# Moving the last expert's third output take one cosine step later, and another order of five small and middle-sized buffers

## The chip, the core and the metric

The kernel runs on one core of one Trainium2 chip. The metric is the device time of one launch in microseconds (us). One core has TensorE (PE, the matrix products; PEld is its weight load), VectorE (DVE), ScalarE (ACT), GpSimd (POOL) and SyncE (SP), which here only issues the loads and the stores. Each engine works through its own list of instructions; where one needs another's result, it waits on a counter (a semaphore).

## What is computed

A windowed attention, then a mixture of four experts, then a feed-forward block with a cosine in it:

```python
scores = q @ k.T / sqrt(D); mask: 0 <= i - j < 64; attn = softmax(scores); x = attn @ v
p = domain_probs / sum(domain_probs)
out = sum over e in 0..3 of p[:, e:e+1] * (relu(x @ w1[e]) @ w2[e])
h = out @ w_in;  g = h * cos(h);  result = g @ w_out
```

There are 1152 tokens of width 512. Each expert has 1024 hidden columns, the last block 2048, worked as two halves of 1024. All is float32.

## The kernel before

**Numbers in two parts.** Every operand of a large product is split into a high and a low part (`x_hi`, `x_lo`, `w_hi`, `w_lo`, `hp_hi`, `hp_lo`), and each product is three matmuls: high by high, high by low, low by high. ACT writes the high parts, DVE the low parts of activations, POOL the low parts of weights.

**Tiles.** Tokens are worked in three tiles of 384 (`TOK`, `NTOK = 3`), hidden columns in eight chunks of 128 (`FC = 8`). An *up* step of a chunk is 12 matmuls of 384 columns at L1153 (4 chunks of the width by 3 products). It reads weights as the stationary operand and x as the moving one, and writes one PSUM bank. A *down* step is 9 matmuls of 512 columns at L1181 (3 groups of 128 tokens by 3 products). It reads `hp_hi` or `hp_lo` as the stationary operand and weights as the moving one, and adds to the three PSUM banks 4, 5 and 6 (`y_ps[0:3]`) over the eight chunks. Experts 1 to 3 do two of their tiles in products of pairs (L1198, L1212, with helpers `t_hi`, `t_lo`, `ex_hi`, `ex_lo`), and the third tile alone with up and down steps.

**Taking outputs.** When all eight down steps of a tile are done, DVE empties the three banks into `acc`. For experts it multiplies by the tokens' shares: `pick_shares` copies three shares per partition from `p_tok` to `p_now` (L874), and `take_shared` does one 512-column instruction per bank (L882 for expert 0, L885 afterwards), each of which raises the counter `y_taken` by one. The first down step of the next tile waits for `y_taken` bank by bank: `down_cells(0, ...)` has `pe.wait_ge(y_taken, y_count(tile, c))` before the three matmuls of each c.

**From the experts to the cosine block.** After the third expert tile of expert 3 (`pe_alone(E - 1)`) PE's list is: up 0 of the cosine block, down 6 of the expert, up 1, down 7 (the last of the expert), up 2, and then, in `pe_turn`, up 3, down 0, up 4, down 1, up 5, down 2 and so on. Down 0 is the first that writes banks 4 to 6 again. Hidden chunks of the cosine block go through bank `f % 4`, and DVE and ACT turn each into h times cos(h) in this chain:

- ACT `cosine`: `c_u` from the bank (L692), then `hidden_high_cos` of the step before (L681), then for some steps `high_weights` (L608), then `c_abs` (L699) and `c_cos` (L701), which reads `half_pi`.
- DVE `times_cosine`: `c_k` (L978), `c_r1` (L980), `c_r2` (L983), `hidden_low_cos` of the step before (L863), then a take if the step has one, then `h_raw` = `c_cos` times the bank (L991).

The three steps 0, 1 and 2 before the turn are written out in a loop of their own (`for i in range(LAG)`, `LAG = 3`), on ACT and on DVE. In step 1 of it DVE also takes the expert's third tile, `take_last_of_experts`: one copy and three takes. POOL meanwhile works eight instructions of 128 columns per chunk of weights (L426).

**Buffers.** `sb(name, shape)` places buffers one behind another in each partition, each start rounded up to a multiple of 32 bytes. `half_pi` is one number per partition, `p_now` nine, `apart` sixteen that nobody reads or writes.

Of the kernel before, what the change touches and what calls it, by code (L numbers as in the profile page):

```python
# [26 lines left out]
P = 128  # L27
# [16 lines left out]
FC = F1 // P  # L44
TOK = 384
NTOK = N // TOK
OC = TOK // P
TILES = N // P
HALVES = F2 // F1
LAG = 3  # L50
# [58 lines left out]
def build(nc, q, k, v, probs, weights, out):  # L109
    with ExitStack() as ctx:  # L110
        def sb(name, shape, dt=F32):
            return ctx.enter_context(nc.sbuf_tensor(name, shape, dt))
# [7 lines left out]
        x_hi = sb("x_hi", [P, DC, N], F32R)  # L120
        x_lo = sb("x_lo", [P, DC, N], F32R)
        p_tok = sb("p_tok", [P, E, TILES])
        half_pi = sb("half_pi", [P, 1])

        sb("apart", [P, 16])
        hp_hi = sb("hp_hi", [P, HP, TOK], F32R)
        hp_lo = sb("hp_lo", [P, HP, TOK], F32R)
        h_raw = sb("h_raw", [P, HP, TOK])
        p_now = sb("p_now", [P, NTOK, OC])
        ident = sb("ident", [P, P])  # L130
        mask = sb("mask", [P, 3, P])
        zeros = sb("zeros", [P, P])
# [138 lines left out]
        MIX = NTOK + E - 1  # L271
# [528 lines left out]
        def _(dve):  # L800
# [60 lines left out]
            def hidden_low_cos(f, s):  # L861
                dve.wait_ge(hp_hi_done, s + 1 + C_HI)
                nc.vector.tensor_tensor(hp_lo[:, f % HP, :], h_raw[:, f % HP, :], hp_hi[:, f % HP, :],  # L863
                                        ALU.subtract).then_inc(hp_lo_done, 1)
# [109 lines left out]
            def times_cosine(f, s, late, take=None, which=()):  # L974
                n = s - MIX * FC
                bank_h = h_ps[f % HB][:, 0:TOK]
                dve.wait_ge(cos_u, n + 1)
                nc.vector.tensor_scalar_sub(c_k, c_u, ROUND).then_inc(cos_k, 1)  # L978
                dve.wait_ge(cos_k, n + 1)
                nc.vector.scalar_tensor_tensor(out=c_r1, in0=c_k, scalar=-TWO_PI_HI, in1=bank_h,  # L980
                                               op0=ALU.mult, op1=ALU.add).then_inc(cos_r1, 1)
                dve.wait_ge(cos_r1, n + 1)
                nc.vector.scalar_tensor_tensor(out=c_r2, in0=c_k, scalar=-TWO_PI_LO, in1=c_r1,  # L983
                                               op0=ALU.mult, op1=ALU.add).then_inc(cos_r, 1)
                if late:
                    hidden_low_cos((f - 1) % FC, s - 1)
                if take is not None:
                    take(*which)
                dve.wait_ge(cos_done, n + 1)
                dve.wait_ge(hp_hi_done, s - HP + 1 + C_HI)  # L990
                nc.vector.tensor_tensor(h_raw[:, f % HP, :], c_cos, bank_h, ALU.mult).then_inc(cos_taken, 1)  # L991

            def dve_turn(e, t, turn, last=False, inputs=False):
                for f in range(FC):
                    g, s = (f + LAG) % FC, turn * FC + f + LAG
                    if last and f >= FC - LAG:
                        if f == FC - LAG:
                            hidden_low_cos(FC - 1, s - 1)
                    elif f < FC - 1:
                        times_cosine(g, s, True)  # L1000
                    else:
                        times_cosine(g, s, True, take_outputs, (e, turn, t))
                    if inputs and f in TURNS:
                        next_input_low((t - 1) % NTOK * OC + TURNS.index(f))
                if last:
                    take_outputs(e, turn, t, last)
# [67 lines left out]
                    take_last_tile(E - 1, c)  # L1074

            for i in range(LAG):
                if i == 1:
                    times_cosine(i, MIX * FC + i, True, take_last_of_experts)
                else:
                    times_cosine(i, MIX * FC + i, i > 0)  # L1080
            dve_turn(E, 0, MIX, inputs=True)
            with dve.Fori(1, NTOK - 1) as t:
                dve_turn(E, t, MIX + t)
# [376 lines left out]
```

## Time and profile before

| | us |
|---|---|
| median of 3 runs | 645.05 |
| lowest, highest | 644.95, 645.10 |
| the profiled execution, its time | 645.05 |
| its span, first to last instruction | 643.0 |
| PE busy in the span | 632.9 |
| DVE, ACT, POOL busy | 306.4, 259.2, 269.6 |

The span leaves out 2.05 us around the instructions. Since the profiled execution took the median time, what is added to or taken from its span is added to or taken from 645.05. Matmuls overlap, so a matmul's own duration is longer than the distance from its start to the next one's start; where the text needs PE's pace, it takes starts.

### The profile page before, as it was taken

To read this page: it belongs to the slowest core of one execution; us is meant where nothing else is said; L and a number is where in the kernel's file an instruction comes from. 1 tells how busy PE (TensorE), PEld (TensorE's weight loads), DVE (VectorE), ACT (ScalarE), POOL (GpSimd) and SP (SyncE) were. 2 spreads that over 40 slices of the span, in tenths; PEclk is the share of its full clock that TensorE was granted. 3 is DMA by queue.
4 is the path that set the end of the run, shared out by engine and by line. 5 is a ranking of instruction groups with operands and counts; after the bars stand their busy time and mean duration, and the time that the engine had idled before them with its cause. 6 is when DMAs were issued, how large, how long until landed. Compare 5 with 4: busy or idle time off the path is not lost.

```text
span 643.0 us, 10145 instructions
## 1 busy us (share of the span) xinstructions
PE 632.9 (98%) x3656; PEld 564.9 (88%) x3656; DVE 306.4 (48%) x722; ACT 259.2 (40%) x554; POOL 269.6 (42%) x404
## 2 busy tenths in 40 slices
PE   7899999999999999999999999999999999999998
PEld 6687889999999999999999999999899999999996
DVE  6655331215433315433415333427775666756674
ACT  6685412233321233321233321246554467555452
POOL 6683336597730187730197730277100059400000
PEclk9999999999999999999999999999999999999999
DMA  9855200003210012210022120043100012001011
GB/s 280 260 185 143 104 1 1 1 19 113 66 67 1 1 65 65 65 65 0 1 65 66 66 66 1 2 128 102 34 0 1 0 41 93 1 0 49 0 50 49
DMA packets 21896, 37.25 MB, mean 58 GB/s; under 512 B 2784, under 2 KB 14048, under 8 KB 21856
## 3 DMA queue, kind: packets, MB, share of 16 engines
q1 hardware_dynamic: 20688, 36.71, 17.7%
q8 instruction: 24, 0.39, 0.2%
q10 hardware_dynamic: 1168, 0.02, 0.1%
q14 instruction: 16, 0.13, 0.1%
HBM read 34.36 MB, written 2.36 MB: 57 GB/s over the span
## 4 chain that ended last, share of the span: by engine, by line
PE 95%; DVE 2%; issue 1%; ACT 1%; POOL 0%; DVEq 0%
PE bank L1181 31%; PE bank L1153 31%; PE bank L1212 15%; PE bank L1198 14%; PE bank L1145 2%; PE bank L1109 1%; PE bank L1129 1%; DVE s_sb L823 1%; PE bank L1295 1%; PE bank L1334 1%; ACT prob L576 0%; DVE acc L972 0%; ACT x_hi L589 0%; DVE p_now L874 0%; DVE prob_t L838 0%
## 5 line engine op out<-in xcount | busy, mean ns | idle before, releaser
L426 POOL TENSOR_TENSOR w_lo<-w_raw,w_hi 128x128 fp32r<-128x128 f32 (+1 forms) x252 | 149.7, 628 | 208.8 <-ACT w_hi L608 206.7
L1153 PE MATMUL bank<-x_hi,w_hi 128*128 128x384 f32 (+1 forms) x384 | 132.2, 344 | 0.2 <-DVE x_lo L852 0.2
L1153 PE MATMUL bank<-x_hi,w_lo 128*128 128x384 f32 (+1 forms) x384 | 129.5, 337 | 0.0
L1153 PE MATMUL bank<-x_lo,w_hi 128*128 128x384 f32 (+1 forms) x384 | 129.1, 336 | 0.0
L1181 PE MATMUL bank<-w_hi,hp_hi 128*128 128x512 f32 x288 | 113.6, 394 | 0.3 <-DVE acc L882 0.3
L1181 PE MATMUL bank<-w_lo,hp_hi 128*128 128x512 f32 x288 | 113.9, 395 | 0.0
L1181 PE MATMUL bank<-w_hi,hp_lo 128*128 128x512 f32 x288 | 113.6, 394 | 0.0
L926 DVE TENSOR_TENSOR h_raw<-bank,h_raw 128x384 f32<-128x384 f32 x84 | 46.8, 557 | 97.2 <-PE bank L1198 97.2
L1153 PEld LDWEIGHTS bank<-x_hi,w_hi 128*128 128x128 f32 x384 | 72.2, 188 | 5.4 <-issue 1.0
L1153 PEld LDWEIGHTS bank<-x_lo,w_hi 128*128 128x128 f32 x384 | 72.2, 188 | 3.3
L632 ACT ACTIVATE hp_hi<-h_raw 128x384 fp32r<-128x384 f32 x48 | 25.3, 527 | 117.6 <-DVE h_raw L926 117.6
L857 DVE SCALAR_TENSOR_TENSOR hp_lo<-bank,hp_hi 128x384 fp32r<-128x384 f32 x48 | 26.5, 556 | 96.8 <-ACT hp_hi L640 54.8
L1153 PEld LDWEIGHTS bank<-x_hi,w_lo 128*128 128x128 f32 x384 | 72.0, 188 | 0.0
L1181 PEld LDWEIGHTS bank<-w_lo,hp_hi 128*128 128x128 f32 x288 | 54.0, 187 | 11.6
L1181 PEld LDWEIGHTS bank<-w_hi,hp_hi 128*128 128x128 f32 x288 | 54.1, 188 | 9.4 <-issue 0.6
L1181 PEld LDWEIGHTS bank<-w_hi,hp_lo 128*128 128x128 f32 x288 | 54.0, 188 | 8.7
L1212 PE MATMUL bank<-w_lo,hp_hi 128*128 128x512 f32 x144 | 56.4, 392 | 0.0
L1212 PE MATMUL bank<-w_hi,hp_lo 128*128 128x512 f32 x144 | 56.4, 391 | 0.0
L1212 PE MATMUL bank<-w_hi,hp_hi 128*128 128x512 f32 x144 | 56.3, 391 | 0.0
L699 ACT ACTIVATE c_abs<-c_r 128x384 f32<-128x384 f32 x48 | 25.3, 527 | 46.2 <-DVE c_r L983 46.1
L608 ACT ACTIVATE w_hi<-w_raw 128x1024 fp32r<-128x1024 f32 x40 | 42.0, 1050 | 0.0
L991 DVE TENSOR_TENSOR h_raw<-c_cos,bank 128x384 f32<-128x384 f32 x48 | 26.6, 553 | 32.4 <-ACT c_cos L701 32.4
(103 smaller groups left out, 965.9 us busy)
## 6 DMA issues: line engine op xcount, KB each, us to landing
w_raw<-in_weights SPq DMA_DIRECT2D x43, 512.0 KB, 3.6
q_t<-in_q SPq DMA_DIRECT2D x12, 192.0 KB, 4.6
result<-acc SPq DMA_DIRECT2D x9, 256.0 KB, 2.0
w_raw<-in_weights SPq DMA_DIRECT2D x8, 256.0 KB, 5.9
k_t<-in_k SPq DMA_DIRECT2D x8, 224.0 KB, 5.3
v_w<-in_v SPq DMA_DIRECT2D x4, 384.0 KB, 4.8
v_w<-in_v SPq DMA_DIRECT2D x4, 320.0 KB, 6.5
k_t<-in_k SPq DMA_DIRECT2D x4, 192.0 KB, 4.0
```

Source lines behind the costliest of these rows:

```text
L426: last = nc.gpsimd.tensor_tensor(w_lo[:, f, at:at + part], raw[:, at - begin:at - begin + part], w_hi[:, f, at:at + part], ALU.subtract)
L608: nc.scalar.activation(w_hi[:, f, :], w_raw[:, f % STAGE, :], ACT.Copy).then_inc(w_hi_done, 1)
L632: nc.scalar.activation(hp_hi[:, i, :], h_raw[:, i, :], ACT.Relu).then_inc(pair_hi_done, 1)
L699: nc.scalar.activation(c_abs, c_r2, ACT.Abs).then_inc(cos_abs, 1)
L857: nc.vector.scalar_tensor_tensor(out=hp_lo[:, f % HP, :], in0=ps[:, 0:TOK], scalar=0.0, in1=hp_hi[:, f % HP, :], op0=ALU.max, op1=ALU.subt ...
L926: nc.vector.tensor_tensor(h_raw[:, place, :], ps, h_raw[:, other, :], ALU.add).then_inc(pair_taken, 1)
L991: nc.vector.tensor_tensor(h_raw[:, f % HP, :], c_cos, bank_h, ALU.mult).then_inc(cos_taken, 1)
L1145: last = nc.tensor.matmul(o_bank(m)[heads, block_of * WIN:(block_of + 1) * WIN], v_w[:, r, WINDOW_OF[t][block_of], heads], prob_t[:, h, bl ...
L1153: last = nc.tensor.matmul(ps[:, 0:TOK], w[:, f, chunk(c)], x[:, c, token_cols(t)], start=c == 0 and i == 0, stop=c == DC - 1 and i == 2)
L1181: last = nc.tensor.matmul(y_ps[c][:, :], h[:, f % HP, chunk(c)], w[:, f, DM:2 * DM], start=f == 0 and i == 0, stop=f == FC - 1 and i == 2)
L1198: last = nc.tensor.matmul(bank[(g * PRODUCTS + j) % 2][:, 0:TOK], a, b, start=c == 0 and i == 0, stop=c == 1 and i == 2)
L1212: last = nc.tensor.matmul(pair_y[t][c][:, :], h[:, i, chunk(c)], w[:, f, DM:2 * DM], start=f == 0 and k == 0, stop=f == FC - 1 and k == 2)
```

## The change

```diff
@@ buffers
         x_lo = sb("x_lo", [P, DC, N], F32R)
         p_tok = sb("p_tok", [P, E, TILES])
-        half_pi = sb("half_pi", [P, 1])
-
-        sb("apart", [P, 16])
+        p_now = sb("p_now", [P, NTOK, OC])
         hp_hi = sb("hp_hi", [P, HP, TOK], F32R)
         hp_lo = sb("hp_lo", [P, HP, TOK], F32R)
         h_raw = sb("h_raw", [P, HP, TOK])
-        p_now = sb("p_now", [P, NTOK, OC])
+        half_pi = sb("half_pi", [P, 1])
         ident = sb("ident", [P, P])
@@ DVE, before the cosine block's first turn
             for i in range(LAG):
-                if i == 1:
+                if i < LAG - 1:
+                    times_cosine(i, MIX * FC + i, i > 0)
+                else:
                     times_cosine(i, MIX * FC + i, True, take_last_of_experts)
-                else:
-                    times_cosine(i, MIX * FC + i, i > 0)
```

**Buffers.** `p_now` now stands between `p_tok` and `hp_hi`, `half_pi` between `h_raw` and `ident`, and `apart` is gone. Worked out from the sizes, the starts in bytes within a partition are:

| buffer | before | after | start modulo 64, before and after |
|---|---|---|---|
| w_hi, w_lo, w_raw, x_hi, x_lo, p_tok | 16512 to 135296 | the same | 0, 0 |
| hp_hi | 135552 | 135520 | 0, 32 |
| hp_lo | 141696 | 141664 | 0, 32 |
| h_raw | 147840 | 147808 | 0, 32 |
| half_pi | 135456 | 153952 | 32, 32 |
| p_now | 153984 | 135456 | 0, 32 |
| ident, mask, zeros, acc and all behind them | 154048 on | 64 less each | unchanged |

**Order.** The take of the last expert's third tile moves from step 1 of the three written-out steps to step 2. This is the only place at which an engine's list differs. In DVE's list, from `c_k` of step 1 on, before:

```order
462 L978 TENSOR_SCALAR c_k<-c_u 128x384 [waits cos_u]
463 L980 SCALAR_TENSOR_TENSOR c_r1<-c_k,bank1 128x384 [waits cos_k]
464 L983 SCALAR_TENSOR_TENSOR c_r2<-c_k,c_r1 128x384 [waits cos_r1]
465 L863 TENSOR_TENSOR hp_lo<-h_raw,hp_hi 128x384 [waits hp_hi_done]
466 L874 COPY p_now<-p_tok 128x3
467 L885 SCALAR_TENSOR_TENSOR acc<-bank4,p_now,acc 128x512 [waits down_done,p_picked]
468 L885 SCALAR_TENSOR_TENSOR acc<-bank5,p_now,acc 128x512
469 L885 SCALAR_TENSOR_TENSOR acc<-bank6,p_now,acc 128x512
470 L991 TENSOR_TENSOR h_raw<-c_cos,bank1 128x384 [waits hp_hi_done,cos_done]
471 L978 TENSOR_SCALAR c_k<-c_u 128x384 [waits cos_u]
```

The same place with the change (its lines stand two lower, since two lines of the buffers are gone):

```order
465 L861 TENSOR_TENSOR hp_lo<-h_raw,hp_hi 128x384 [waits hp_hi_done]
466 L989 TENSOR_TENSOR h_raw<-c_cos,bank1 128x384 [waits hp_hi_done,cos_done]
467 L976 TENSOR_SCALAR c_k<-c_u 128x384 [waits cos_u]
468 L978 SCALAR_TENSOR_TENSOR c_r1<-c_k,bank2 128x384 [waits cos_k]
469 L981 SCALAR_TENSOR_TENSOR c_r2<-c_k,c_r1 128x384 [waits cos_r1]
470 L861 TENSOR_TENSOR hp_lo<-h_raw,hp_hi 128x384 [waits hp_hi_done]
471 L872 COPY p_now<-p_tok 128x3
472 L883 SCALAR_TENSOR_TENSOR acc<-bank4,p_now,acc 128x512 [waits down_done,p_picked]
473 L883 SCALAR_TENSOR_TENSOR acc<-bank5,p_now,acc 128x512
474 L883 SCALAR_TENSOR_TENSOR acc<-bank6,p_now,acc 128x512
475 L989 TENSOR_TENSOR h_raw<-c_cos,bank2 128x384 [waits hp_hi_done,cos_done]
```

So the copy and the three takes now stand behind `c_k` of step 2, which waits for `cos_u` of step 2. In PE's list the end of up 3 and down 0 of the cosine block are the instructions that wait for these takes; they read, in the kernel before:

```order
1754 L1153 MATMUL bank3<-x_hi,w_lo 128x384
1755 L1181 MATMUL bank4<-w_hi,hp_hi 128x512 [waits y_taken,hp_lo_done]
1756 L1181 MATMUL bank4<-w_hi,hp_lo 128x512
1757 L1181 MATMUL bank4<-w_lo,hp_hi 128x512
1758 L1181 MATMUL bank5<-w_hi,hp_hi 128x512 [waits y_taken]
```

and with the change:

```order
1754 L1151 MATMUL bank3<-x_hi,w_lo 128x384
1755 L1179 MATMUL bank4<-w_hi,hp_hi 128x512 [waits y_taken,hp_lo_done]
1756 L1179 MATMUL bank4<-w_hi,hp_lo 128x512
1757 L1179 MATMUL bank4<-w_lo,hp_hi 128x512
1758 L1179 MATMUL bank5<-w_hi,hp_hi 128x512 [waits y_taken]
```

Nothing moved on PE, nor on ACT, POOL or SP.

## Rows read from the trace of the kernel before

**Rows 1.** The page: busy time of the engines, and the chain that ended last.

```profile
PE 632.9 (98%) x3656; PEld 564.9 (88%) x3656; DVE 306.4 (48%) x722; ACT 259.2 (40%) x554; POOL 269.6 (42%) x404
...
PE 95%; DVE 2%; issue 1%; ACT 1%; POOL 0%; DVEq 0%
```

**Rows 2.** Stretches A:B: length, then busy us of each engine, PEclk, DMA, GB/s.

```profile
442.00:514.00 72.00, 72.00 (x371) 65.57 (x370) 50.85 (x100) 39.02 (x75) 8.24 (x16) 1.00 0.07 22
514.00:580.00 66.00, 66.00 (x333) 59.72 (x332) 44.80 (x85) 40.10 (x72) 31.30 (x64) 1.00 0.10 33
```

**Rows 3.** Timeline of PE, up 2, up 3, down 0: start, us, what, idle before.

```profile
441.70 0.33 PE L1153 MATMUL bank<-x_hi,w_hi 128*128 128x384 f32 x1
...
443.81 0.33 PE L1153 MATMUL bank<-x_hi,w_hi 128*128 128x384 f32 x1
...
445.88 0.39 PE L1181 MATMUL bank<-w_hi,hp_hi 128*128 128x512 f32 x1
```

**Rows 4.** Timeline of DVE, steps 0 to 2 of the cosine block.

```profile
436.15 0.36 DVE L978 TENSOR_SCALAR c_k<-c_u 128x384 f32<-128x384 f32 x1 [1.31 <-ACT c_u L692]
...
440.69 0.48 DVE L978 TENSOR_SCALAR c_k<-c_u 128x384 f32<-128x384 f32 x1
441.20 0.56 DVE L980 SCALAR_TENSOR_TENSOR c_r<-c_k,bank 128x384 f32<-128x384 f32 x1
441.80 0.56 DVE L983 SCALAR_TENSOR_TENSOR c_r<-c_k,c_r 128x384 f32<-128x384 f32 x1
442.27 0.55 DVE L863 TENSOR_TENSOR hp_lo<-h_raw,hp_hi 128x384 fp32r<-128x384 f32 x1
442.74 0.43 DVE L874 COPY p_now<-p_tok 128x3 f32<-128x3 f32 x1
443.20 2.07 DVE L885 SCALAR_TENSOR_TENSOR acc<-bank,p_now,acc 128x512 f32<-128x512 f32 x3
445.19 0.55 DVE L991 TENSOR_TENSOR h_raw<-c_cos,bank 128x384 f32<-128x384 f32 x1
445.65 0.66 DVE L978 TENSOR_SCALAR c_k<-c_u 128x384 f32<-128x384 f32 x1
446.34 0.56 DVE L980 SCALAR_TENSOR_TENSOR c_r<-c_k,bank 128x384 f32<-128x384 f32 x1
...
447.41 0.82 DVE L863 TENSOR_TENSOR hp_lo<-h_raw,hp_hi 128x384 fp32r<-128x384 f32 x1
```

**Rows 5.** Timeline of ACT and of POOL, steps 0 to 2.

```profile
435.63 0.49 ACT L692 ACTIVATE c_u<-bank 128x384 f32<-128x384 f32 x1 [1.51 <-PE bank L1153]
...
442.95 0.62 ACT L701 ACTIVATE c_cos<-c_abs,half_pi 128x384 f32<-128x384 f32 x1
444.00 0.49 ACT L692 ACTIVATE c_u<-bank 128x384 f32<-128x384 f32 x1 [0.44 <-PE bank L1153]
445.77 0.53 ACT L681 ACTIVATE hp_hi<-h_raw 128x384 fp32r<-128x384 f32 x1 [1.27 <-DVE h_raw L991]
...
442.36 3.73 POOL L426 TENSOR_TENSOR w_lo<-w_raw,w_hi 128x128 fp32r<-128x128 f32 x8 [1.41 <-ACT w_hi L608]
```

**Rows 6.** Timeline of PE and of DVE, expert 0: a down step waits for a take.

```profile
87.57 0.34 PE L1153 MATMUL bank<-x_hi,w_lo 128*128 128x384 f32 x1
88.22 0.47 PE L1181 MATMUL bank<-w_hi,hp_hi 128*128 128x512 f32 x1 [0.31 <-DVE acc L882]
88.52 0.40 PE L1181 MATMUL bank<-w_hi,hp_lo 128*128 128x512 f32 x1
88.75 0.40 PE L1181 MATMUL bank<-w_lo,hp_hi 128*128 128x512 f32 x1
88.99 0.39 PE L1181 MATMUL bank<-w_hi,hp_hi 128*128 128x512 f32 x1
...
87.32 2.07 DVE L882 TENSOR_SCALAR acc<-bank,p_now 128x512 f32<-128x512 f32 x3
```

**Rows 7.** Timeline of DVE where POOL is idle: a cosine step, and a copy of shares.

```profile
519.12 0.36 DVE L978 TENSOR_SCALAR c_k<-c_u 128x384 f32<-128x384 f32 x1 [0.84 <-ACT c_u L692]
519.51 0.55 DVE L980 SCALAR_TENSOR_TENSOR c_r<-c_k,bank 128x384 f32<-128x384 f32 x1
520.10 0.56 DVE L983 SCALAR_TENSOR_TENSOR c_r<-c_k,c_r 128x384 f32<-128x384 f32 x1
520.58 0.82 DVE L863 TENSOR_TENSOR hp_lo<-h_raw,hp_hi 128x384 fp32r<-128x384 f32 x1
...
208.54 0.16 DVE L874 COPY p_now<-p_tok 128x3 f32<-128x3 f32 x1
```

**Rows 8.** Groups of PE's weight loads: busy us, mean ns of one.

```profile
L1181 PEld LDWEIGHTS bank<-w_hi,hp_hi 128*128 128x128 f32 x288 | 54.1, 188 | 9.4 <-issue 0.6
```

## The prediction, made before the changed kernel ran

> **What bounds the kernel now.** I read the page first. TensorE is busy for 632.9 of 643.0 us and holds 95% of the chain that ended last; the other engines are busy for less than half of the span [rows 1]. So a step on another engine counts only where PE comes to wait for it. Next I asked which stretches have any idle time of PE left. From 442 us on there is none: 72.00 busy of 72.00 us, then 66.00 of 66.00 [rows 2]. That matters twice. A new wait of PE in this part adds its full length, since nothing behind it can shrink; and a faster DVE or ACT there gains nothing. Then I went to the place that the change touches, with the timelines of PE, DVE and ACT side by side [rows 3 to 5]. The reader should look for two moments: when PE starts down 0 of the cosine block (445.88), and when DVE starts the three takes that this down step waits for (443.20).
>
> **How much cover the take has now.** Down 0 needs the first take. What lies between them is seen in one other place of the trace, where PE really waited for a take: the takes began at 87.32 and the matmul behind them at 88.22, 0.90 us later [rows 6]. So a take that starts at 443.20 lets down 0 start at 444.10, and it starts at 445.88. The cover is 1.78 us: the take may slip by that much for nothing, and beyond it each microsecond is PE's.
>
> **By how much it slips.** In the changed list the copy and the takes stand behind `c_k`, `c_r1`, `c_r2` and `hp_lo` of step 2, and `c_k` of step 2 waits for ACT's `c_u` of step 2. That one cannot move: ACT started it at 444.00 after idling for PE's up 2 [rows 5], and up 2 runs in both kernels at 441.70 to 443.81 [rows 3]. So the start of the new chain is fixed by PE itself, and the freed time of DVE in step 1 does not pull it forward. Step by step:
>
> - `c_u` starts at 444.00. In step 0, where DVE idled for `c_u`, `c_k` started 0.52 after it (435.63 to 436.15) [rows 4, 5]. So `c_k` of step 2 starts at 444.52. DVE is free by then: `c_cos` of step 1 is done at 443.57, `h_raw` takes 0.55 from there to about 444.15. ACT's `hp_hi` of step 1 needs this `h_raw` and the end of `c_u` (444.49), and is done at about 445.05; `hp_lo` wants it at 446.1, so it is in time.
> - From `c_k` to the first take the same five instructions ran in step 1 in 0.51 + 0.60 + 0.47 + 0.47 + 0.46 = 2.51 us (440.69 to 443.20) [rows 4]. The first take starts at 444.52 + 2.51 = 447.03.
> - The matmul of down 0 follows 0.90 later, at 447.93 [rows 6].
> - It started at 445.88, so PE stands for **2.05 us**. In other words, a slip of 3.83 us (443.20 to 447.03) less the cover of 1.78.
>
> The second and third banks add nothing: takes follow each other at 0.69 us (2.07 for three), and where PE waited before, its next bank came 0.77 after the first (88.22 to 88.99) [rows 6].
>
> **What queues behind it.** On DVE, `h_raw` of step 2 stands behind the takes. It starts at 447.03 + 1.99 (443.20 to 445.19) = 449.02 [rows 4]; `hp_lo` of step 2 follows after `c_k`, `c_r1`, `c_r2` of step 3, 0.46 + 0.51 + 0.60 + 0.47 later, at 451.1, and is done by 451.9 even at the longer 0.82. PE needs it at down 2. Between down 0 and down 2 stand down 0, up 4, down 1 and up 5, each 2.07 to 2.11 (441.70, 443.81, 445.88) [rows 3], so down 2 comes at 447.93 + 8.4 = 456.3. Four microseconds are left, and the second wait does not arise. ACT and POOL are behind DVE and PE here and are asked for nothing earlier.
>
> **Bounds of this term.** Low end: POOL does not disturb DVE at all. A cosine step then ran 0.39 + 0.59 + 0.48 to `hp_lo`, and the copy took 0.16 in place of 0.43 [rows 7]; with 0.47 from `hp_lo` to the copy and about 0.19 for the copy, the chain is 2.12, and PE stands 1.66 us. High end: `c_k` is held as in step 2 of before (445.65 to 446.34, 0.69 in place of 0.51) and `hp_lo` takes 0.82 in place of 0.55 [rows 4]; the chain is 2.96 and PE stands 2.50 us. POOL is at work until 446.09 [rows 5] and ACT can give it its next chunk about 1.2 us earlier than now, so some disturbance is likely, as in step 1, where POOL was working when the copy came; I keep 2.05.
>
> The rule behind these holds is in the Trainium skill, SBUF — State Buffer, section Who interferes with whom: a DVE instruction with two SBUF inputs, or in a two-port mode, and a GpSimd instruction that reads SBUF exclude each other for a whole instruction. The trace agrees: the copy of three numbers took 0.43 beside a working POOL and 0.16 without. By this rule alone, the result lies between the two bounds and not below.
>
> **The buffers.** No instruction is added or removed by them. Only `hp_hi`, `hp_lo`, `h_raw` and `p_now` change their place within 64 bytes. PE reads `hp_hi` and `hp_lo` only as weights. Such a load takes 188 ns [rows 8], while matmuls of a down step start 0.23 apart (88.52, 88.75) [rows 6], and loads run beside them. So a load could grow by some 40 ns before PE saw it. On DVE and ACT the writers of these buffers lie in steps that have room (DVE idled 0.84 before `c_k` in one) [rows 7]. No row shows a large buffer at an odd multiple of 32 bytes, so its price is bounded, not read: I take zero. Down to where it could help, see the third rival.
>
> In the Trainium skill, SBUF — State Buffer, section The DMA port swizzle, SBUF lines are 16 bytes long; every start here is a multiple of 32, so by that rule a shift by 32 or 64 is free and 647.1 stands. No run here shows it yet.
>
> **The sum.** 645.05 + 2.05 + 0 = **647.1 us**, 0.32% more. The bounds give 646.7 and 647.6. About 0.2%, or 1.29 us, is what a measurement of this kernel can tell from no change.
>
> **Rivals.**
>
> *Longer loads of shifted weights.* If a load from an odd multiple of 32 bytes took more than the 230 ns between matmuls, each nanosecond above would cost 432 x 3 = 1296 of them 1.3 us (288 and 144 per product, at L1181 and L1212). A load one eighth longer would take 211 ns and cost nothing; one a quarter longer, 235 ns, would cost 5 ns x 1296 = 6.5 us: 653.6. For it speaks only that such a start is not in the trace. Against it: it decides only above 1.22 times the present load. Chance 0.03.
>
> *The take is not late enough (not slower).* The mechanism is the cover: PE stands only if the first take starts later than 444.98, and the cost stays below 1.29 if it starts before 446.27. From `c_k` at 444.52 that leaves 1.75 for a chain whose quickest form is 2.12. It would need `c_u` of step 2 to come over 0.4 earlier, and that hangs on PE's up 2. If it did so the time would be 645.1 to 646.3. Also here: down 0 might in fact be released by an earlier count. In the code it waits for all takes up to this tile, so I give it little. Chance 0.08.
>
> *The new places give PE something back (faster).* Up steps that follow a down step take 2.11 (441.70 to 443.81), the one that follows an up step 2.07 (443.81 to 445.88) [rows 3]. If the 0.04 came from where buffers stand and went away in some 90 up steps, 3.6 us would be won: 645.05 + 2.05 - 3.6 = 643.5. It decides the sign from 52 of these steps on (2.05 / 0.04), and the 0.2% from 84 on ((2.05 + 1.29) / 0.04). Against it: both steps read the same buffers, and what differs is what stands before them. Chance 0.04.
>
> *A longer wait.* POOL or ACT disturb the chain beyond the upper bound, for example each of the three takes is held too: 647.6 to 648.5. Chance 0.05.
>
> **How the numbers follow.** The forecast with its bounds has 0.80. Slower by over 0.2%: 0.80 + 0.05 + 0.03 = 0.88. Within 0.2%: 0.08. Faster: 0.04. The range must hold 0.80; I take it a little wider than the two bounds, 646.5 to 647.9, for the spread of runs (0.15 us) and part of the longer wait.
>
> **What would show it.** In the profile of the changed kernel: (1) PE idles before the first matmul of down 0 for about 1.8 to 2.1 us, put down to `acc`, DVE L883, and at no other new place; (2) `c_u` of step 2 still starts at about 444.0; (3) the three takes start at about 447.0; (4) the span is about 645.1; (5) weight loads stay at 188 ns and down steps at their pace. The forecast is wrong if down 0 starts at 445.9 as before, if the idle time is there and the span is not longer (then PE caught up somewhere, against rows 2), or if the matmuls' pace has changed everywhere.

## The result and the profile after

The changed kernel takes **651.88 us** (median of four, 650.37 to 652.26) beside 645.0 for the kernel before (four, 644.86 to 645.1): a ratio of 1.0102, with an interval of 1.0085 to 1.012. So it is slower, as forecast, but by 6.9 us where the forecast had 2.05, and outside the range of 646.5 to 647.9. Its profiled execution took 650.12 us, with a span of 648.2 (643.0 before). These 5.2 us can be read from the trace; the timed executions took up to 2.1 us more than the profiled one.

The page of the changed kernel, busy time and chain, against [rows 1]:

```profile
PE 635.3 (98%) x3656; PEld 564.0 (87%) x3656; DVE 305.9 (47%) x722; ACT 258.5 (40%) x554; POOL 269.0 (41%) x404
...
PE 95%; DVE 3%; issue 1%; ACT 1%; POOL 0%; DVEq 0%
```

PE has the same 3656 matmuls and is busy for 2.4 us more; the span grew by 5.2. So there is a wait, and there is work that became longer. The waits of PE (line, what for: us in total, times, longest) have one new entry, the one that was forecast:

```profile
PE bank L1179 <- DVE acc L883: 2.1, 1, 2.1
```

The timelines of PE (last matmul of up 3, start of down 0) and of DVE (step 2), against [rows 3] and [rows 4]:

```profile
447.61 0.34 PE L1151 MATMUL bank<-x_hi,w_lo 128*128 128x384 f32 x1
450.07 0.47 PE L1179 MATMUL bank<-w_hi,hp_hi 128*128 128x512 f32 x1 [2.12 <-DVE acc L883]
```

```profile
446.43 0.46 DVE L976 TENSOR_SCALAR c_k<-c_u 128x384 f32<-128x384 f32 x1 [0.42 <-ACT c_u L690]
446.93 0.55 DVE L978 SCALAR_TENSOR_TENSOR c_r<-c_k,bank 128x384 f32<-128x384 f32 x1
447.51 0.56 DVE L981 SCALAR_TENSOR_TENSOR c_r<-c_k,c_r 128x384 f32<-128x384 f32 x1
447.99 0.81 DVE L861 TENSOR_TENSOR hp_lo<-h_raw,hp_hi 128x384 fp32r<-128x384 f32 x1
448.72 0.41 DVE L872 COPY p_now<-p_tok 128x3 f32<-128x3 f32 x1
449.17 0.75 DVE L883 SCALAR_TENSOR_TENSOR acc<-bank,p_now,acc 128x512 f32<-128x512 f32 x1
```

ACT's `c_u`, for which this `c_k` waited, and POOL's work beside it:

```profile
445.90 0.49 ACT L690 ACTIVATE c_u<-bank 128x384 f32<-128x384 f32 x1 [0.48 <-PE bank L1151]
```

```profile
444.22 7.82 POOL L424 TENSOR_TENSOR w_lo<-w_raw,w_hi 128x128 fp32r<-128x128 f32 x16 [1.41 <-ACT w_hi L606]
```

The reader is to see that the chain is the forecast one, link for link, but 1.90 us later in the program: `c_u` starts at 445.90 in place of 444.00, and PE ends up 3 just as much later. So something had slowed PE down before the edited step was reached.

**Where the 5.2 us lie.** Three moments of PE cut the span into pieces that both kernels share: the first down step of the second tile of expert 0 (88.22 in [rows 6]; "the first down step" below), down 0 of the cosine block (445.88 in [rows 3]), and the last matmul. The first and the last of them in the changed kernel, and the last of the kernel before:

```profile
87.62 0.47 PE L1179 MATMUL bank<-w_hi,hp_hi 128*128 128x512 f32 x1 [0.29 <-DVE acc L880]
...
644.65 0.40 PE L1179 MATMUL bank<-w_lo,hp_hi 128*128 128x512 f32 x1
```

```profile
639.41 0.39 PE L1181 MATMUL bank<-w_lo,hp_hi 128*128 128x512 f32 x1
```

| piece | before | after | difference |
|---|---|---|---|
| start of the span to the first down step | 88.22 | 87.62 | -0.60 |
| first down step to where down 0 would follow up 3 | 357.66 | 360.16 | +2.50 |
| the wait ahead of down 0 | 0 | 2.29 | +2.29 |
| down 0 to the last matmul | 193.53 | 194.58 | +1.05 |
| sum | 639.41 | 644.65 | +5.24 |

(Up 3's last matmul starts at 447.61; in [rows 3] matmuls of up 3 pass into down 0 at the same pace, 0.17 apart, so down 0 would have come at 447.78. It came at 450.07.) What comes ahead of it holds the loads, the attention and the first tile, and varies from execution to execution: in the traces of this study the first down step lies between 87.38 and 88.27. So the wait is worth 2.29 us, and 3.55 us come from matmuls that follow each other more slowly, in places where no instruction of the order was changed. The middle piece was measured in the same way for every kernel below; for the five kernels in which all of these buffers stand to each other as before, it agrees to 0.02 us once the wait is taken off, so it tells a pace more sharply than the median of the runs.

### The profile page after: what moved, and what is told of

Read it like the earlier page. It is cut to its first block, busy times and chain, and to the rows that moved or that the text cites. A ratio compares the mean times of both kernels' runs of the same rounds, so it can differ in the third digit from the quotient of the medians.

```text
span 648.2 us, 10145 instructions
## 1 busy us (share of the span) xinstructions
PE 635.3 (98%) x3656; PEld 564.0 (87%) x3656; DVE 305.9 (47%) x722; ACT 258.5 (40%) x554; POOL 269.0 (41%) x404
## 4 chain that ended last, share of the span: by engine, by line
PE 95%; DVE 3%; issue 1%; ACT 1%; POOL 0%; DVEq 0%
PE bank L1179 31%; PE bank L1151 30%; PE bank L1210 16%; PE bank L1196 14%; PE bank L1143 2%; PE bank L1107 1%; PE bank L1127 1%; DVE s_sb L821 1%; PE bank L1293 1%; PE bank L1332 1%; ACT prob L574 0%; DVE acc L970 0%; DVE p_now L872 0%; DVE w_hi L846 0%; ACT x_hi L587 0%
## 5 line engine op out<-in xcount | busy, mean ns | idle before, releaser
L1179 PE MATMUL bank<-w_hi,hp_hi 128*128 128x512 f32 x288 | 115.7, 402 | 2.4 <-DVE acc L883 2.1
L1210 PE MATMUL bank<-w_hi,hp_hi 128*128 128x512 f32 x144 | 57.1, 396 | 0.0
```

The costliest lines, as they stand in the source:

```text
L1179: last = nc.tensor.matmul(y_ps[c][:, :], h[:, f % HP, chunk(c)], w[:, f, DM:2 * DM], start=f == 0 and i == 0, stop=f == FC - 1 and i == 2)
L1210: last = nc.tensor.matmul(pair_y[t][c][:, :], h[:, i, chunk(c)], w[:, f, DM:2 * DM], start=f == 0 and k == 0, stop=f == FC - 1 and k == 2)
```

## The experiments

**The two halves of the change.** `layout_only` has the new buffers and the take in step 1; `take_only` has the old buffers and the take in step 2.

```diff
 layout_only:
-        half_pi = sb("half_pi", [P, 1])
-
-        sb("apart", [P, 16])
+        p_now = sb("p_now", [P, NTOK, OC])
...
-        p_now = sb("p_now", [P, NTOK, OC])
+        half_pi = sb("half_pi", [P, 1])
 take_only:
-                if i == 1:
+                if i < LAG - 1:
+                    times_cosine(i, MIX * FC + i, i > 0)
+                else:
                     times_cosine(i, MIX * FC + i, True, take_last_of_experts)
-                else:
-                    times_cosine(i, MIX * FC + i, i > 0)
```

> Only the buffers of the change; the take stays in step 1. In the changed kernel's profile the matmuls that load hp_hi or hp_lo as weights start about 4 to 7 ns further apart, and PE's span grew by 3.1 us beside the 2.1 us wait. Theory P (the new places slow PE's pace): ratio about 1.005 to 1.008 (648.2 to 650 us), no new wait of PE. Rival S (the take's step explains all, the pace is chance between executions): 645.0, ratio within 1.001.

> Only the take moved to step 2; the buffers stay. Theory P: 647.1 (ratio 1.003), PE waits 2.1 us at the first down step of the cosine block and its pace is that of before. Rival S: 650 to 652, with runs as scattered as those of the changed kernel. Rival C (the wait costs more than its length in the timed runs, since their granted clock was 0.997 where the profiled run had 1.0): 648 to 649.

Measured: `layout_only` 648.21 us (ratio 1.0057, 1.004 to 1.0073), `take_only` 648.28 (1.0059, 1.0041 to 1.0076), each beside 644.88. So +3.3 and +3.4, together 6.7 of the 6.9. Both halves cost, and neither needs the other. In `layout_only` PE starts the first down step and down 0 here:

```profile
87.45 0.48 PE L1179 MATMUL bank<-w_hi,hp_hi 128*128 128x512 f32 x1 [0.29 <-DVE acc L880]
...
447.63 0.40 PE L1179 MATMUL bank<-w_hi,hp_hi 128*128 128x512 f32 x1
```

That is 360.18 in place of 357.66, with no wait in it: +2.52, and +1.00 from there to the end. The pace is the buffers'. `take_only` has 357.67 up to where down 0 would follow, as before to 0.01, and a wait:

```profile
444.98 0.34 PE L1153 MATMUL bank<-x_hi,w_lo 128*128 128x384 f32 x1
447.48 0.47 PE L1181 MATMUL bank<-w_hi,hp_hi 128*128 128x512 f32 x1 [2.16 <-DVE acc L885]
447.79 0.39 PE L1181 MATMUL bank<-w_hi,hp_lo 128*128 128x512 f32 x1
...
448.97 0.63 PE L1181 MATMUL bank<-w_lo,hp_hi 128*128 128x512 f32 x1
449.40 0.63 PE L1181 MATMUL bank<-w_hi,hp_hi 128*128 128x512 f32 x1
...
450.68 0.52 PE L1153 MATMUL bank<-x_hi,w_hi 128*128 128x384 f32 x1
```

The wait cost 447.48 - 445.15 = 2.33 us. But behind it matmuls stand 0.43 apart (448.97, 449.40) where they stood 0.23 apart before. The stretches of this trace (length, busy us of PE, PEld, DVE, ACT, POOL, then PEclk, the granted clock) say why:

```profile
446.00:447.00 1.00, 0.00 (x0) 0.00 (x0) 0.96 (x3) 0.97 (x3) 1.00 (x3) 1.00 0.28 45
447.00:448.00 1.00, 0.52 (x2) 0.49 (x3) 1.00 (x3) 0.07 (x1) 1.00 (x3) 1.00 0.54 152
448.00:449.00 1.00, 1.00 (x5) 0.73 (x4) 1.00 (x2) 0.00 (x0) 1.00 (x4) 0.70 0.80 328
449.00:450.00 1.00, 1.00 (x4) 0.81 (x3) 0.97 (x3) 0.52 (x1) 0.43 (x2) 0.50 0.00 0
...
452.00:453.00 1.00, 1.00 (x8) 1.00 (x7) 0.55 (x1) 0.04 (x1) 0.00 (x0) 1.00 0.30 119
```

PE idled, worked again at the full clock for under a microsecond, and then had the lower of the two levels, 0.50 or 1.2 GHz, before it came back to 2.4. From down 0 to the last matmul this kernel needs 195.15 us, 1.62 more than before. So a wait of 2.33 us cost 3.95 us in this execution. The four executions took 648.17, 649.55, 648.39 and 647.38, with mean granted clocks of 0.997, 0.995, 0.997 and 1.0; the one at 1.0 is 2.5 above the kernel before, about the wait alone. The mean alone doesn't show such a fall, though: the profiled execution of `swap_only`, a kernel without the wait that comes further down, has 0.997 as well, from 0.68 between 10 and 15 us, and its span is 642.4.

**Does the clock fall because PE idles?** `filled_wait` is `take_only` with twelve matmuls of 384 columns between up 3 and down 0, into a bank that nobody needs then. The take is as late as in `take_only`, but PE works through most of the time.

```diff
+                    if inputs and f == 0:
+                        pe.wait_ge(x2_lo_done, 2 * OC)
+                        for _ in range(12):
+                            nc.tensor.matmul(y_ps[3][:, 0:TOK], w_hi[:, LAG, chunk(0)], x_hi[:, 0, token_cols(0)],
+                                             start=True, stop=True)
```

> take_only with twelve extra matmuls of 384 columns (w_hi and x_hi into PSUM bank 7, which nobody reads before it is written anew) between up 3 and down 0, where PE waited for 2.16 us in take_only; they are 12 x 0.174 = 2.09 us long, so the wait for the take is as long but PE works through it. The extra work isn't part of the reference. Theory G (the wait lets the granted clock fall to 1.2 GHz for about 3.3 us behind it, and that is the second half of take_only's 3.3 us): no stretch at 0.5 there, 647.1 (ratio 1.0032). Rival D (the late take delays something behind it, or the cosine steps are slower, whatever PE does): 648.3 as take_only.

Measured: 647.23 us (646.66 to 647.59), ratio 1.0038 (1.0023 to 1.0052) beside 644.81: +2.4. The extra matmuls and down 0, and the stretch around them:

```profile
445.24 2.24 PE L1313 MATMUL bank<-x_hi,w_hi 128*128 128x384 f32 x12
447.58 0.47 PE L1181 MATMUL bank<-w_hi,hp_hi 128*128 128x512 f32 x1
```

```profile
442.00:452.00 10.00, 9.90 (x54) 9.23 (x53) 8.10 (x15) 5.76 (x11) 7.56 (x16) 1.00 0.40 129
```

Down 0 comes as late as in `take_only` (359.99 behind the first down step, there 360.00), yet the clock stays at 1.00, and the rest takes 193.60 us, 0.07 more than before. So the useful work is delayed by 2.34 us and nothing else is lost. With the idle PE `take_only` lost 1.62 us more in its trace and 648.28 - 647.23 = 1.05 more in the medians. That the clock falls because PE idles is likely by this, but not shown: each kernel has one trace, the changed kernel's trace has the same idle time and keeps 1.00, and the intervals of the two ratios overlap (1.0041 to 1.0076, 1.0023 to 1.0052).

**Which buffers set the pace?** First the small ones against the large ones. `swap_only` exchanges `half_pi` and `p_now` as the change does, with paddings that leave all large buffers where they were; `hp_by_32` moves `hp_hi`, `hp_lo` and `h_raw` 32 bytes down, nothing else.

```diff
 swap_only:
-        half_pi = sb("half_pi", [P, 1])
-        sb("apart", [P, 16])
+        p_now = sb("p_now", [P, NTOK, OC])
+        sb("apart", [P, 8])
...
-        p_now = sb("p_now", [P, NTOK, OC])
+        half_pi = sb("half_pi", [P, 1])
+        sb("behind", [P, 8])
 hp_by_32:
-        sb("apart", [P, 16])
+        sb("apart", [P, 8])
...
         h_raw = sb("h_raw", [P, HP, TOK])
+        sb("behind", [P, 8])
```

> p_now and half_pi stand where the change puts them by their neighbours, with unused numbers beside them so that every other buffer keeps its start of before; the take stays. Theory P1: 645.0, ratio within 1.001. Rival P3 (small buffers next to hp_hi and h_raw disturb): 648 to 650.

> hp_hi, hp_lo and h_raw start 32 bytes lower (apart has 8 numbers in place of 16, and 8 unused numbers follow h_raw), every other buffer stays where it is in before, and the take too. Theory P1 (the weight operand's own start, at an odd multiple of 32, sets the pace): as layout_only, 648 to 650. Rival P2 (what counts is the shift by 64 bytes of t_hi, t_lo, ex_hi, ex_lo, acc and the rest): 645.0 here. Rival P3 (the neighbours p_now and half_pi): 645.0 here.

Measured: `swap_only` 644.88 (ratio 1.0001, 0.9991 to 1.001), `hp_by_32` 648.22 (1.0052, 1.0035 to 1.0069). The small buffers do nothing; the 32 bytes of the three large ones are nearly all of it (3.44 us of the 3.52 of `layout_only`, in the table below).

Then one buffer at a time, `hp_hi` 32 bytes lower, `hp_lo` or `h_raw` 32 bytes higher, with paddings that leave the rest where it was (`hp_hi_by_32`) or move what stands behind by 128 bytes (the other two):

```diff
 hp_hi_by_32:
-        sb("apart", [P, 16])
+        sb("apart", [P, 8])
         hp_hi = sb("hp_hi", [P, HP, TOK], F32R)
+        sb("behind", [P, 8])
 hp_lo_by_32:
         hp_hi = sb("hp_hi", [P, HP, TOK], F32R)
+        sb("apart1", [P, 8])
         hp_lo = sb("hp_lo", [P, HP, TOK], F32R)
+        sb("apart2", [P, 24])
 h_raw_by_32:
         hp_lo = sb("hp_lo", [P, HP, TOK], F32R)
+        sb("apart1", [P, 8])
         h_raw = sb("h_raw", [P, HP, TOK])
+        sb("apart2", [P, 24])
```

> Only hp_hi starts 32 bytes lower; hp_lo, h_raw and all else as before. hp_hi is the weight operand of two of three matmuls in a down step. Theory P1 (a weight load from an odd multiple of 32 is what slows PE, per load): 2/3 of hp_by_32's 3.3 us, 647.1 (ratio 1.0035). Rival P4 (only the load that stands at a change from one buffer to the other is slow): all or nothing, 648.2 or 645.0. Rival P5 (h_raw's place, on DVE and ACT, is the cause): 645.0.

> Only hp_lo starts 32 bytes off (higher); h_raw and all behind it start 128 bytes higher. Theory R: down steps pay in part, as with hp_hi_by_32 (645.6) or more, since the sum of hp_by_32 (3.3 us) isn't reached by hp_hi alone (0.8): 645.5 to 647.5. If single loads added up, 644.9 + 3.3 - 0.8 = 647.4; if it depends on the pair, the time may also be near 645.

> h_raw alone starts 32 bytes later; hp_hi and hp_lo stay, and what stands behind moves by 128 bytes. TensorE never reads h_raw. Theory (the pace is set by the places of TensorE's own operands): same as before, 644.9, first down step to down 0 of the cosine block 357.66 us, down 0 to the last matmul 193.5 us. Rival (h_raw takes part, through the banks that DVE and ACT use beside TensorE): hp_hi alone and hp_lo alone stretched the two parts together by 0.73 and 1.63 us, all three by 3.44 us, so h_raw would have the other 1.1 us: 645.9 or more.

Measured: 645.63 (1.0013, 1.0003 to 1.0023), 646.16 (1.0024, 1.0014 to 1.0033) and 644.43 (0.9993, 0.9983 to 1.0002). By the pieces of PE they cost +0.73, +1.63 and -0.36 us, where all three together cost +3.44. None of the three expectations for `hp_hi_by_32` fits. The rival that `h_raw` carries the missing 1.1 fell, but the theory beside it missed as well: it forecast 357.66 for the first piece, and 357.35 was measured. That need not be `h_raw`, which PE never reads: the helpers of the pairs (`t_hi`, `t_lo`, `ex_hi`, `ex_lo`) stand behind it and moved by 128 bytes, and PE reads them in the first piece only; the second is 193.48 beside 193.53. No run separates the two.

The sum +0.73 + 1.63 - 0.36 = 2.00 isn't a clean test of whether the effects add, since `hp_lo` and `h_raw` moved up where `hp_by_32` moved them down, and 128 bytes came in behind them. The steps of PE show more. An up step is timed from its first matmul to the first of the down step behind it, a down step likewise. These are down 1, up 5 and down 2 in the kernel before, down 1, up 5 and down 2 in the changed one, and the same in `hp_hi_by_32`:

```profile
450.07 0.39 PE L1181 MATMUL bank<-w_hi,hp_hi 128*128 128x512 f32 x1
452.15 0.33 PE L1153 MATMUL bank<-x_hi,w_hi 128*128 128x384 f32 x1
454.26 0.39 PE L1181 MATMUL bank<-w_hi,hp_hi 128*128 128x512 f32 x1
```

```profile
454.33 0.40 PE L1179 MATMUL bank<-w_hi,hp_hi 128*128 128x512 f32 x1
456.43 0.33 PE L1151 MATMUL bank<-x_hi,w_hi 128*128 128x384 f32 x1
458.54 0.40 PE L1179 MATMUL bank<-w_hi,hp_hi 128*128 128x512 f32 x1
```

```profile
450.34 0.40 PE L1182 MATMUL bank<-w_hi,hp_hi 128*128 128x512 f32 x1
452.44 0.33 PE L1154 MATMUL bank<-x_hi,w_hi 128*128 128x384 f32 x1
454.52 0.40 PE L1182 MATMUL bank<-w_hi,hp_hi 128*128 128x512 f32 x1
```

These lengths are steady through the cosine block. With the change a down step takes 2.10 in place of 2.08, and the up step stays at 2.11. With `hp_hi` alone the down step takes the same 2.10, so the theory of two thirds of the loss fell; but the up step takes 2.08. Over the whole kernel that is +3.11 us in the down steps and -2.35 in the up steps (table below). An up step reads neither `hp_hi` nor `hp_lo`, so the place of a buffer also acts on steps that don't read it. Why is open.

Then whether it is a buffer's own start, or how the starts stand to each other. `all_by_32` moves everything up by 32 bytes; `hp_by_64` moves the three large ones 64 bytes down; `rest_by_64` moves every large buffer except these three by 64 bytes.

```diff
 all_by_32:
+        sb("ahead", [P, 8])
         w_hi = sb("w_hi", [P, FC, 2 * DM], F32R)
 hp_by_64:
-        sb("apart", [P, 16])
...
         h_raw = sb("h_raw", [P, HP, TOK])
+        sb("behind", [P, 16])
 rest_by_64:
+        sb("ahead", [P, 16])
         w_hi = sb("w_hi", [P, FC, 2 * DM], F32R)
...
-        sb("apart", [P, 16])
...
         h_raw = sb("h_raw", [P, HP, TOK])
+        sb("behind", [P, 16])
```

> Eight unused numbers ahead of w_hi: every buffer of the kernel starts 32 bytes higher, so their distances to each other are those of before and all stand at an odd multiple of 32. Theory P1 (each load by its own start): down steps lose as in hp_by_32, and up steps, whose weight operand is w_hi or w_lo, lose too: 648 to 652. Rival P7 (what counts is the place of the weight operand against that of the moving one): 645.0.

> hp_hi, hp_lo and h_raw start 64 bytes lower (apart is gone and 16 unused numbers follow h_raw), all else as before, so they stand at an even multiple of 32 but at an odd one of 64. Theory P1 with a grain of 64 bytes: 644.9, no loss. Rival P6 (a grain of 128 bytes, or any distance to the other operands' phase): 646.5 to 648.2.

> hp_hi, hp_lo and h_raw stand where they do in before; every other large buffer (w_hi, w_lo, w_raw, x_hi, x_lo, acc, t and ex) starts 64 bytes higher. Theory R (only the place of TensorE's operands against each other counts, modulo 128): the same as hp_by_64, 643.2 (ratio 0.9975). Rival A (hp's own place counts): 644.9, ratio within 1.001.

Measured: 644.81 (1.0, 0.9991 to 1.001), 643.15 (0.9975, 0.9964 to 0.9987) and 642.71 (0.9969, 0.9957 to 0.998). With everything moved by 32 bytes, PE's pieces are the old ones: the first down step at 87.38 and down 0 at 445.04 are 357.66 apart.

```profile
87.38 0.47 PE L1182 MATMUL bank<-w_hi,hp_hi 128*128 128x512 f32 x1 [0.31 <-DVE acc L883]
...
445.04 0.39 PE L1182 MATMUL bank<-w_hi,hp_hi 128*128 128x512 f32 x1
```

So the theory that a start at an odd multiple of 32 bytes is slow in itself fell. And `hp_by_64` and `rest_by_64`, which share only the 64 bytes between the two sets of buffers, have the same pieces (356.84 and 192.64; 356.85 and 192.64): what counts is how the buffers stand to each other. Both expectations for `hp_by_64`, no change and a loss, fell too: it is faster than the kernel before, by 0.82 us in the first piece and 0.89 in the second.

**A version that beats both.** `no_apart` is the kernel before without its padding line; `hp_x_by_64` moves in addition `x_hi` and `x_lo` by 64 bytes.

```diff
 no_apart:
-        sb("apart", [P, 16])
 hp_x_by_64: the same, and
         w_raw = sb("w_raw", [P, STAGE, 2 * DM])
+        sb("ahead_x", [P, 16])
         x_hi = sb("x_hi", [P, DC, N], F32R)
         x_lo = sb("x_lo", [P, DC, N], F32R)
+        sb("behind_x", [P, 16])
```

> The line with apart is left out, nothing else: hp_hi, hp_lo, h_raw and everything behind them start 64 bytes lower. Theory R: the gain of hp_by_64 in the down steps (1.7 us) and a change of some tenths in the pairs' products, whose t and ex now stand at 0 against w, x: 643 to 643.8. Rival (the gain of hp_by_64 came with the small buffers behind): 644.9.

> As no_apart, and x_hi and x_lo at 64 modulo 128 as well, against w_hi and w_lo at 0. In before an up step behind a down step has four matmuls of 176 to 185 ns among those of 173. Theory R: the up steps' pace moves too, by -0.04 to +0.1 us a step over some 90 steps: 640 to 652, and not the time of no_apart. Rival (only operands of 512-column matmuls are sensitive): as no_apart.

Measured: `no_apart` **643.12 us** (642.76 to 643.26), ratio 0.997 (0.9959 to 0.9981), 1.7 us faster than the kernel before and 8.8 faster than the changed one. `hp_x_by_64` 645.44 (1.0011, 1.0002 to 1.0021). The gain of the first piece is gone and more. Against the kernel before its down steps, which don't read x, lose 2.71 us, where those of `no_apart` win 1.68, and its up steps win 1.85 (table below). This doesn't show that the place of x counts: with the 128 bytes put in around x, `hp_hi` and `hp_lo` stand 64 bytes further from the weights than in the kernel before, and in `no_apart` 64 bytes nearer. No run moves these two sets by 128 bytes and nothing else, so the place of x and these 128 bytes stand as rivals.

**Where the pace shows, and where it doesn't.** The table has both pieces for each kernel (the first from the first down step to down 0, the second from there to the last matmul), each from three rows of its PE timeline, and the change of their sum. For `take_only`, `filled_wait` and the changed kernel the wait is left out of the first piece. In the second of these the extra matmuls stand in its place. The last two columns divide that sum between the kinds of steps, by the distance from the start of each of their matmuls to the next one's start (down steps 281.97 us in the kernel before, up steps 266.04, both with the products of pairs); between kernels of equal distances they scatter by 0.1. The wait is left out of the up steps as well.

| kernel | first piece | second piece | sum against before | median less before | of it in down steps | in up steps |
|---|---|---|---|---|---|---|
| before | 357.66 | 193.53 | | |  |  |
| `swap_only` | 357.66 | 193.52 | -0.01 | 0.0 | -0.09 | +0.07 |
| `all_by_32` | 357.66 | 193.52 | -0.01 | 0.0 | -0.11 | +0.10 |
| `take_only` | 357.67 | 195.15 | +1.63 | +3.4 with the wait | +1.08 | +0.55 |
| `filled_wait` | 357.65 | 193.60 | +0.06 | +2.4 with the wait | -0.04 | +0.10 |
| `h_raw_by_32` | 357.35 | 193.48 | -0.36 | -0.4 | -0.28 | -0.08 |
| `hp_hi_by_32` | 358.46 | 193.46 | +0.73 | +0.8 | +3.11 | -2.35 |
| `hp_lo_by_32` | 358.88 | 193.94 | +1.63 | +1.3 | +1.83 | -0.22 |
| `hp_by_32` | 360.03 | 194.60 | +3.44 | +3.3 | +3.29 | +0.15 |
| `layout_only` | 360.18 | 194.53 | +3.52 | +3.3 | +3.50 | +0.02 |
| after | 360.16 | 194.58 | +3.55 | +6.9 with the wait | +3.51 | +0.02 |
| `hp_x_by_64` | 358.69 | 193.38 | +0.88 | +0.6 | +2.71 | -1.85 |
| `hp_by_64` | 356.84 | 192.64 | -1.71 | -1.7 | -1.27 | -0.44 |
| `rest_by_64` | 356.85 | 192.64 | -1.70 | -2.2 | -1.23 | -0.48 |
| `no_apart` | 356.82 | 192.68 | -1.69 | -1.7 | -1.68 | 0.00 |

So what the change loses by its buffers, and what `no_apart` gains, is lost and gained in the down steps, whose weights are `hp_hi` and `hp_lo`. `hp_hi` alone loses as much there, but wins 2.35 us in the up steps. The groups of PE by form show it faintly. These are groups of matmuls of down steps (busy us, mean ns of one | idle before) in the kernel before, in the changed one and in `no_apart`:

```profile
L1181 PE MATMUL bank<-w_hi,hp_hi 128*128 128x512 f32 x288 | 113.6, 394 | 0.3 <-DVE acc L882 0.3
L1181 PE MATMUL bank<-w_lo,hp_hi 128*128 128x512 f32 x288 | 113.9, 395 | 0.0
L1212 PE MATMUL bank<-w_hi,hp_hi 128*128 128x512 f32 x144 | 56.3, 391 | 0.0
```

```profile
L1179 PE MATMUL bank<-w_hi,hp_hi 128*128 128x512 f32 x288 | 115.7, 402 | 2.4 <-DVE acc L883 2.1 <-DVE acc L880 0.3
L1179 PE MATMUL bank<-w_lo,hp_hi 128*128 128x512 f32 x288 | 113.9, 396 | 0.0
L1210 PE MATMUL bank<-w_hi,hp_hi 128*128 128x512 f32 x144 | 57.1, 396 | 0.0
```

```profile
L1180 PE MATMUL bank<-w_hi,hp_hi 128*128 128x512 f32 x288 | 114.4, 397 | 0.3 <-DVE acc L881 0.3
L1180 PE MATMUL bank<-w_lo,hp_hi 128*128 128x512 f32 x288 | 112.0, 389 | 0.0
L1211 PE MATMUL bank<-w_hi,hp_hi 128*128 128x512 f32 x144 | 56.6, 393 | 0.0
```

With the change the mean matmul of `w_hi` by `hp_hi` is 8 ns longer at one line and 5 ns at the other, and the second product at the first line by 1 ns; in `no_apart` one product is slower than before and another faster, and the sum is in its favour. So the pace isn't the same for all products, and no single load explains it. The weight loads of the changed kernel, against [rows 8], show nothing of it:

```profile
L1179 PEld LDWEIGHTS bank<-w_hi,hp_hi 128*128 128x128 f32 x288 | 54.1, 188 | 11.5 <-issue 3.0
```

What inside the chip makes two operands disturb each other was not shown. Two reads of PE, the weights of the next matmul and the moving columns of this one, that meet in the same part of the memory would fit: such a clash depends on both starts and vanishes from the sum when all move together. That stays an argument, and by itself it doesn't say why an up step becomes faster when only `hp_hi` moves. Offsets finer than 32 bytes weren't tried, nor `x` or the weights alone.

## Why the prediction was right in its direction and wrong in its size

**The cover and the slip: right.** The chain from `c_u` to down 0 has three terms. `c_u` to `c_k`: forecast 0.52, measured 0.53 (445.90 to 446.43). `c_k` to the first take: forecast 2.51, measured 2.74 (446.43 to 449.17). Take to matmul: forecast 0.90 from an expert's down step, measured 0.90 (449.17 to 450.07), and again 0.90 in `take_only` (446.58 to 447.48). Their sum, less the 1.88 by which PE would have followed `c_u` in both kernels, is 2.05 forecast and 2.29 measured, inside the bounds of 1.66 and 2.50.

**The term that was a little short.** The 0.23 us come from one place: from `hp_lo` to the copy it took 0.73 (447.99 to 448.72) where step 1 had 0.47; the other links together gave 0.03 back. The prediction named it, a held `hp_lo` of 0.82, but as the high end. It wrote that ACT can give POOL its next chunk earlier; that happened, and POOL's row shows sixteen instructions without a gap from 444.22 on, where before it had eight, from 442.36, and stopped at 446.09 [rows 5]. The freed ACT fed POOL sooner, and POOL then stood beside the very chain that had become critical. The value should have been taken with POOL busy throughout.

**No second wait: right.** PE's waits have one new entry and no other.

**"A new wait adds its full length, since nothing behind it can shrink": too little.** Nothing behind it shrank, but in `take_only`'s trace something grew: PE's clock fell after the idle time. That cost 1.62 us there, and the medians with and without the idle PE are 1.05 apart. In the profiled execution of the changed kernel it didn't happen; matmuls behind the wait stand 0.23 apart there. Its timed executions took 0.25 to 2.1 us more than the profiled one, the size that such a fall has in `take_only`, but no trace of those exists. The median of 651.88 is 1.8 above the profiled execution, and 1.0 above 645.0 + 2.29 + 3.55. So for these last 1 to 1.8 us of the 6.9 the clock is the likely cause and not a shown one; the 1.0 is also within what the interval of the ratio leaves open (5.5 to 7.7 us). The prediction read the granted clock, 1.00 in both stretches [rows 2], and never asked what an idle PE would do to it.

**"I take zero" for the buffers: wrong, and the largest error.** It cost 3.3 us alone (`layout_only`), 3.55 in the trace of the changed kernel. The step that failed is the one from the length of a weight load to the pace of the matmuls: "a load could grow by some 40 ns before PE saw it". The load did not grow at all (188 before, 188 after), so both this step and the rival of longer loads looked at a number that is blind to the effect. PE is not paced by the recorded load; the starts of matmuls moved while every recorded load stayed. The prediction also called the price "bounded, not read", and then gave it no width in the range, only rivals with chances of 0.03 and 0.04: no row had two operands at another distance, so it should have stood in the range on both sides. The runs put that range at -1.7 to +3.5 us for shifts of 32 and 64 bytes, wider than all other terms together.

The Trainium skill, SBUF — State Buffer, section The DMA port swizzle, has SBUF lines of 16 bytes. No run here tests that length. What failed is the prediction's inference from it, that a shift by 32 bytes is free: for TensorE's operands it cost 3.3 us, and the measurement decides.

**The rival of new places** had the right kind of quantity, a few hundredths of a microsecond on many steps, at a chance of 0.04, but not what this layout does: its up steps stay at 2.11, and its down steps grow from 2.08 to 2.10. What it described does exist: `hp_hi_by_32` has up steps of 2.08. And its sign was open: 64 bytes gave 1.7 us back. It should have had a mirror image among the cases of slower.

**What the prediction said would show it wrong** did so. It wrote that it would be wrong "if the matmuls' pace has changed everywhere", and the idle time of 2.1 us beside a span longer by 5.2 sent the reading to the pace at once. It had changed in the down steps (+3.51), and hardly in the up steps (+0.02).

## What to carry to other kernels

Where PE is the bound and never idle, a padding or an exchange of buffers is a change of PE's pace until a run says otherwise: here 32 bytes between operands cost 0.5% and 64 gained 0.3%, with no instruction changed, so time a change of order and its change of layout apart. Measure a pace between two named matmuls, first and last of the same work, since the recorded lengths of loads don't show it. And price a new wait of a busy PE at its length, and set the high end of the range for the time that PE may then run at the lower clock (1.6 us in one trace here, nothing in another).

## What the runs showed of the hardware

- **Placement of PE's operands.** With the same instructions, the time from the first down step to down 0 is 357.66 us before, 360.2 with `hp_hi`, `hp_lo` and `h_raw` 32 bytes nearer to the weights and to x, and 356.8 with them 64 bytes nearer; kernels with the same distances repeat it to about 0.02 us. A down step takes 2.08, 2.10 and 2.06 in the cosine block, while each of its weight loads is recorded at 187 or 188 ns. Moved all together by 32 bytes, nothing changes.
- **A buffer acts on steps that don't read it.** `hp_hi` alone 32 bytes lower makes a down step 0.02 us longer, as all three buffers do, and an up step behind a down step 0.03 shorter (2.11 to 2.08), so that in all it costs 0.73 us where the three cost 3.44.
- **The clock.** After 2.2 us of idle time and some further work at 1.00, the granted clock fell to 0.50 in one trace and stayed at 1.00 in another with the same wait. With PE kept at work through most of it, it stayed at 1.00 too.
- **POOL beside DVE.** `hp_lo` took 0.81 us where it began amid POOL's work, against 0.55 in step 1 before, where it began 0.09 before POOL did (442.27 and 442.36 in [rows 4] and [rows 5]). The copy of three numbers took 0.41, and 0.43 in that step, against 0.16 without POOL. The `hp_lo` of 0.82 in [rows 7] isn't one without POOL: POOL began at 520.53 there, 0.05 before it.
